# Choosing experts during a recurrence, four tiles at a time, in a fused attention and mixture-of-experts kernel

## The reference

```python
for t in range(S):                                   # attention, B 4, H 8, S 768, D 48
    state = alpha[:, :, t, :, None] * state + k_t (outer) v_t
    y[:, :, t] = q_t @ state
x = y as (3072 tokens, 384)
logits = unit(x) @ unit(expert_emb).T / tau          # 8 experts
e = argmax(logits);  gate = softmax(logits)[e]
x = gate * (relu(x @ w1[e]) @ w2[e])                 # 384 -> 1024 -> 384, one expert per token
h = x @ w_in;  g = max(0.01 * h, h)                  # 384 -> 2048
out = g @ w_out                                      # 2048 -> 384
```

## Time and profile before

| | |
|---|---|
| median of 3 runs | 880.02 us (879.15 to 881.05) |
| profiled execution | 880.55 us |
| its span, first to last instruction | 878.7 us |
| TensorE busy | 836.8 us, 95% |
| VectorE, ScalarE, GpSimd busy | 419.7, 334.2, 160.1 us |
| mean granted TensorE clock | 0.973 of full |

### The profile page before, as it was taken

One profiled execution on the slowest core, in us unless ns is written; L12 is line 12 of the kernel. 1 busy time (PEld: TensorE's weight loads), 2 busy tenths in 40 slices (PEclk: granted clock), 3 DMA queues, 4 the chain that ended last, 5 costly groups with the idle time before them and its releaser, 6 DMA issues.

```text
span 878.7 us, 17061 instructions
## 1 busy us (share of the span) xinstructions
PE 836.8 (95%) x5435; PEld 751.6 (86%) x5436; DVE 419.7 (48%) x643; ACT 334.2 (38%) x624; POOL 160.1 (18%) x216
## 2 busy tenths in 40 slices
PE   7999974899999999999997999999999999999998
PEld 6888854699999999999985999998998999999997
DVE  7788849444455253455244343343343343343332
ACT  2455443334435344444333333333333333333323
POOL 5566623222222222322210000000000000000000
PEclk7999995899999999999998999999999999999999
DMA  9898860552453351553305000200200300100100
GB/s 220 200 215 207 198 207 0 180 180 65 159 179 123 103 179 32 192 179 105 106 2 107 1 1 25 49 1 6 66 0 0 72 0 0 37 1 1 37 1 36
DMA packets 45265, 76.24 MB, mean 87 GB/s; under 512 B 16231, under 2 KB 35731, under 8 KB 45232
## 3 DMA queue, kind: packets, MB, share of 16 engines
q1 hardware_dynamic: 41264, 64.98, 26.6%
q0 software_dynamic: 3968, 10.82, 3.5%
HBM read 61.63 MB, written 15.53 MB: 88 GB/s over the span
## 4 chain that ended last, share of the span: by engine, by line
PE 84%; issue 4%; DVE 4%; POOL 3%; DMA 2%; SPq 1%; ACT 0%; POOLq 0%; DVEq 0%
PE bank L1326 23%; PE bank L1319 23%; PE bank L1269 15%; PE bank L1249 14%; PE bank L1260 3%; POOL kt L522 1%; PE bank L1240 1%; DVE decay L788 1%; PE bank L1148 1%; PE bank L1133 1%; PE bank L1168 1%; DMA xg<-x_rows,isrc 1%; DVE inv L796 1%; POOL state L530 1%; DMA taus<-tau 1%
## 5 line engine op out<-in xcount | busy, mean ns | idle before, releaser
L1319 PE MATMUL bank<-yT,wts 128*128 128x512 f32 x864 | 217.0, 396 | 6.1 <-DVE yT L1082 6.1
L1326 PE MATMUL bank<-wts,gs 128*128 128x384 f32 x1152 | 217.3, 337 | 0.0
L1326 PEld LDWEIGHTS bank<-wts,gs 128*128 128x128 f32 x1152 | 204.4, 188 | 8.9 <-issue 0.4
L1319 PEld LDWEIGHTS bank<-yT,wts 128*128 128x128 f32 x864 | 161.9, 189 | 36.6 <-DVE yT L1082 6.9
L1100 DVE TENSOR_TENSOR g<-bank,small 128x512 f32<-128x512 f32 x96 | 66.4, 691 | 180.6 <-ACT small L743 180.6
L1249 PE MATMUL bank<-wts,gxT 128*128 (+1 forms) x558 | 143.2, 401 | 1.2 <-DVE gxT L1037 1.2
L1269 PE MATMUL bank<-wts,hT 128*128 x744 | 137.3, 339 | 1.6 <-DVE hT L1053 1.6
L1269 PEld LDWEIGHTS bank<-wts,hT 128*128 128x128 f32 x744 | 128.5, 188 | 1.9 <-issue 1.8
L743 ACT ACTIVATE small<-bank 128x512 f32<-128x512 f32 x96 | 57.3, 597 | 191.0 <-PE bank L1319 190.9
L1249 PEld LDWEIGHTS bank<-wts,gxT 128*128 128x128 f32 x558 | 103.0, 190 | 20.9 <-DVE gxT L1037 1.5
L1102 DVE TENSOR_TENSOR gs<-g,gs 128x512 fp32r<-128x512 f32 x96 | 66.4, 692 | 67.0 <-ACT gs L746 67.0
(11 more groups left out here) (155 smaller groups left out, 676.9 us busy)
## 6 DMA issues: line engine op xcount, KB each, us to landing
raw<-w SPq DMA_DIRECT2D x14, 1536.0 KB, 7.1
qkas<-qka SPq DMA_DIRECT2D x40, 289.5 KB, 4.8
vs<-v SPq DMA_DIRECT2D x24, 192.0 KB, 4.7
x_rows<-xs SPq DMA_DIRECT2D x24, 192.0 KB, 4.5
yl<-y_rows SPq DMA_DIRECT2D x24, 192.0 KB, 4.4
out<-os SPq DMA_DIRECT2D x5, 768.0 KB, 4.3
raw<-w_in SPq DMA_DIRECT2D x2, 1536.0 KB, 6.8
raw<-w_out SPq DMA_DIRECT2D x2, 1536.0 KB, 7.3
```

The source lines that it names most:

```text
L1319: m = pe.matmul(gps[f % 2][:, :], wts[:, 0, w_part, n:n + P], yT[:, u, y_part, k], start=(k == 0 and (w_part, y_part) == (0, 0)), stop=(k ...
L1326: m = pe.matmul(ops[tt], gs[:, f % 4, g_part, tt * P:(tt + 1) * P], wts[:, 1, w_part, f * D:(f + 1) * D], start=(f == 0 and (g_part, w_par ...
```

## The change

The loops of the recurrence are written out. After every four tiles (two and two for the last four) VectorE chooses the experts (`route`), TensorE adds up the ranks (`rank_group`) and VectorE turns them into places (`rank`): the place of a token is 3072 times its expert's number plus its rank. GpSimd then scatters the token numbers of one tile with an indirect DMA of 4 byte elements to the DRAM tensor `lists` (`list_ids`), which SyncE filled with the number 3072 (nobody) at the start. The one-hot products and the slot tables are gone.

After 16 tiles one expert must have at least 256 tokens. It is picked (`choose_first`), its weights are loaded first, and its first two blocks come first; the order of experts is rotated to begin with it. GpSimd reads 128 numbers of the list with a DMA, waits for them and gathers with them (`read_ids`, `fetch`), for two blocks in step 21 and for every later block in `take_rows`. Four columns of numbers are used in turn, so reading one waits for the scatter of the block four before. `lay_out` makes the table of blocks while the first two blocks are under way. The gates are worked out after them (`weigh`) and are applied at the end, as the scale of ScalarE's output copy; `take_y` copies `ys` unscaled. Tile n is now row block n of `x_rows`, and the output is written back in the order of the reference. `SURE` is 4, `TILES` 24, `BATCHES` 4, `CH` 6. On VectorE `link` makes the next instruction wait for the one just issued.

```diff
+        GROUP_AT = {BATCHES * (g + 1) + 1: g for g in range(CH - 1)}
...
+            sp.wait_ge(tables_made, 1)
+            sp.dma_start(lists.rearrange("(p n) a -> p (n a)", p=P), nobody[:, :]).then_inc(lists_clear, 16)
...
+                refill_qka(n + 2)
+                if n == TILES - BATCHES - 2:
+                    sp.wait_ge(first_known, 1)
+                    expert0 = sp.value_load(est[0:1, 0:1], min_val=0, max_val=E - 1)
+                if n >= TILES - BATCHES - 2:
+                    load_first(2 * (n - TILES + BATCHES + 2), expert0)
+                    load_first(2 * (n - TILES + BATCHES + 2) + 1, expert0)
...
+            load_first(4, expert0)
+            load_first(5, expert0)
...
+            def list_ids(n, groups):
+                pool.wait_ge(pos_ready, groups)
+                pool.indirect_dma_start(
+                    out=lists, out_offset=bass.IndirectOffsetOnAxis(ap=posi[:, n:n + 1].bitcast(U32), axis=0),
+                    in_=token[:, n:n + 1], in_offset=None, bounds_check=E * CAP - 1, oob_is_err=False).then_inc(id_stored, 16)
...
+            def wait_stored(tiles):
+                pool.wait_ge(id_stored, 16 * tiles)
+                for s in x_stored:
+                    pool.wait_ge(s, 16 * tiles // BATCHES)
...
+            def read_ids(at, j, number):
+                pool.dma_start(members[:, j:j + 1], lists[ds(at, P)]).then_inc(members_in, 16)
+                pool.wait_ge(members_in, number * 16)
                 pool.sem_inc(pool_turns, 1)
...
-            def gather(w, u, n):
-                copy_index(n, isrc, slot_src, w, u)
+            def fetch(j, rows):
+                u = j % 2
                 pool.indirect_dma_start(
-                    out=xg[:, u, :], out_offset=None, in_=x_dram,
-                    in_offset=bass.IndirectOffsetOnAxis(ap=isrc[:, u:u + 1].bitcast(U32), axis=0),
-                    bounds_check=N - 1, oob_is_err=False).then_inc(gathered[u], 16)
...
+                    out=xg[:, u, :], out_offset=None, in_=x_dram[0:rows],
+                    in_offset=bass.IndirectOffsetOnAxis(ap=members[:, j:j + 1].bitcast(U32), axis=0),
+                    bounds_check=rows - 1, oob_is_err=False).then_inc(gathered[u], 16)
...
+            for n in range(TILES):
+                if n + 2 < TILES:
+                    prepare(n + 2)
...
+                if n == SURE * BATCHES + 5:
+                    wait_stored(SURE * BATCHES)
+                    pool.wait_ge(first_known, 1)
+                    expert0 = pool.value_load(est[0:1, 0:1], min_val=0, max_val=E - 1)
+                    for w in range(2):
+                        read_ids(expert0 * CAP + w * P, w, w + 1)
+                        fetch(w, EARLY)
+                if late == 0:
+                    pool.wait_ge(tables_made, TABLES)
+                    pool.wait_ge(lists_clear, 16)
+                if 0 <= late < TILES - BATCHES - 2:
+                    list_ids(late, late // BATCHES + 1)
+                if n == TILES - 2:
+                    list_ids(late + 1, CH - 1)
+                    list_ids(late + 2, CH - 1)
+                if 0 < n <= TILES - BATCHES:
+                    scale_state(n - 1)
+            for n in range(TILES - BATCHES, TILES):
+                list_ids(n, CH + (n - TILES + BATCHES) // 2)
+            wait_stored(TILES)
...
+            def take_rows(w, j, number):
+                at = pool.value_load(wlist[0:1, ds(w, 1)], min_val=0, max_val=E * CAP - P)
+                read_ids(at, j, number)
+                fetch(j, N)
...
-            def step(w, u, nxt, nxt2):
-                nxt3 = not isinstance(w, int) or w + 3 < WINDOWS
+            take_rows(2, 2, 3)
+            def step(w, j, first, nxt3):
                 if nxt3:
                     pool.wait_ge(gx_turned, w + 2)
-                    gather(w + 3, 1 - u, w * 2 + 4)
-                wait_scattered(pool, w, u, pool_turns)
-                copies = w * 2 + 5 if nxt3 else WINDOWS + 1 + w
-                copy_index(copies, idst, slot_dst, w, u)
+                    if not first:
+                        wait_scattered(pool, w + 1, 1 - j % 2)
+                    take_rows(w + 3, (j + 3) % IDS, w + 4)
                 pool.wait_ge(ys_ready, w + 1)
                 pool.sem_inc(pool_turns, 1)
                 pool.indirect_dma_start(
-                    out=y_dram, out_offset=bass.IndirectOffsetOnAxis(ap=idst[:, u:u + 1].bitcast(U32), axis=0),
-                    in_=ys[:, u, :], in_offset=None, bounds_check=N - 1, oob_is_err=False).then_inc(scattered[u], 16)
...
+                    out=y_dram, out_offset=bass.IndirectOffsetOnAxis(ap=members[:, j:j + 1].bitcast(U32), axis=0),
+                    in_=ys[:, j % 2, :], in_offset=None, bounds_check=N - 1, oob_is_err=False).then_inc(scattered[j % 2], 16)
...
+                if n >= FIRST_HI:
+                    split_hi(act, 0, 0, [n - FIRST_HI])
...
+            def route(g):
+                tiles = group_tiles(g)
...
+                dve.wait_ge(lg_copied, tiles[-1] + 1)
+                dve.tensor_reduce(lg, lgq[:, r0:r0 + G], AX.X, ALU.add).then_inc(lg_summed, 1)
...
+                last = len(group_tiles(g - 1)) if g > 0 else 0
+                source = sums[last][:, :, last] if g > 0 else carry[:, :]
+                dve.tensor_copy(heads[G][:, :, 0], source)
+                dve.wait_ge(lg_summed, g + 1)
+                link(dve.tensor_reduce(top, lg, AX.X, ALU.max))
+                link(dve.tensor_tensor(some, lg, over(top), ALU.is_equal))
+                link(dve.tensor_tensor(some, some, prio[:, :].unsqueeze(1).to_broadcast([P, G, E]), ALU.mult))
+                link(dve.tensor_reduce(most, some, AX.X, ALU.max))
+                link(dve.tensor_tensor(heads[G][:, :, 1:].rearrange("p e c -> p c e"), some, over(most), ALU.is_equal))
+                dve.tensor_tensor_scan(flat(sums[G][:, :, :]), flat(marks[G][:, :, :]), flat(heads[G][:, :, :]), 0.0,
+                                       ALU.mult, ALU.add).then_inc(hot_ready, 1)
+            def rank(g):
+                tiles = group_tiles(g)
+                G, n0 = len(tiles), tiles[0]
+                if g < SURE:
+                    dve.wait_ge(tile_done, BATCHES * (g + 1) + 2)
+                else:
+                    dve.wait_ge(rank_ready, g - SURE + 1)
+                ranks = rankps(g == CH)[:, 0:E * G].rearrange("p (e c) -> p e c", e=E)
+                dve.tensor_tensor(hits[G][:, :, :], ranks, heads[G][:, :, 1:], ALU.mult).then_inc(ranked, 1)
+                dve.wait_ge(ranked, g + 1)
+                link(dve.tensor_reduce(best[:, 0:G], hits[G][:, :, :].rearrange("p e c -> p c e"), AX.X, ALU.add))
...
+            def choose_first():
...
+                dve.wait_ge(counts_ready, 1)
+                link(dve.tensor_tensor(have, countps(False), ebase[:, 0, :], ALU.subtract))
+                dve.sem_inc(counted, 1)
+                link(dve.tensor_reduce(most, have, AX.X, ALU.max))
+                link(dve.scalar_tensor_tensor(out=chance, in0=have, scalar=most, in1=prio[:, :],
+                                              op0=ALU.is_equal, op1=ALU.mult))
+                link(dve.tensor_reduce(lead, chance, AX.X, ALU.max))
+                dve.tensor_scalar(est[:, :], lead, -1.0, float(E), ALU.mult, ALU.add).then_inc(first_known, 1)
+            def lay_out():
...
+                dve.wait_ge(first_known, 1)
+                expert0 = dve.value_load(est[0:1, 0:1], min_val=0, max_val=E - 1)
...
+                dve.wait_ge(counts_ready, 2)
+                link(dve.tensor_tensor(wend[:, :], countps(True)[0:1], ebase[0:1, 0, :], ALU.subtract))
...
+                link(dve.tensor_reduce(at, wprod[:, :, :], AX.X, ALU.add))
+                dve.scalar_tensor_tensor(out=wlist[:, :], in0=at, scalar=begin[:, 0:1], in1=wrow[:, :], op0=ALU.add,
+                                         op1=ALU.add).then_inc(tables_ready, 1)
+                link(dve.tensor_reduce(expert, wexp[:, :, :], AX.X, ALU.add))
...
+                link(dve.scalar_tensor_tensor(out=code, in0=second, scalar=4.0 * E, in1=code, op0=ALU.mult, op1=ALU.add))
+                dve.tensor_copy(wtab[:, :], code).then_inc(tables_ready, 1)
...
+            def weigh():
...
+                dve.wait_ge(exp_done, 1)
+                link(dve.tensor_reduce(gsum[:, :], ex[:, :, :], AX.X, ALU.add))
+                link(dve.tensor_scalar(gsum[:, :], gsum[:, :], 1e-9, None, ALU.add))
+                link(dve.reciprocal(gate[:, TG:], gsum[:, :]))
...
+            def take_y(w, u):
+                wait_scattered(dve, w, u)
+                dve.wait_ge(ye_ready, w + 2)
+                dve.tensor_copy(ys[:, u, :], yeps).then_inc(ys_ready, 1)
...
+                if n in GROUP_AT:
+                    route(GROUP_AT[n])
+                if n < TILES - BATCHES:
+                    advance(n)
+                if n in GROUP_AT:
+                    rank(GROUP_AT[n])
+                if n == SURE * BATCHES + 1:
```

(71 more changed lines are left out.)

836 lines of the change are left out of this document (355 added, 481 removed).

## The result

The kernel after takes **960.63 us** (median of 4 runs, 959.36 to 962.76), the kernel before, run beside it, 880.06. The ratio is 1.0918 (95% interval 1.0895 to 1.0941): slower, as forecast, but by 80 us in place of 24, and far outside the range of 876 to 926. The profiled execution has a span of 957.8 us, 79.1 more than before.

What follows compares the result with a forecast made beforehand. TensorE bounds the expert and dense stages, a ring of state, decay, reciprocal, inv and kt the recurrence. 36.2 - 2 + 5.0 - 17.4 + 2 = +23.8 on a span of 878.7 gave 904 us; 8-in-10 range 876 to 926.

Steps and rivals of the forecast that it cites:

- Block loop: Expert blocks: the longer chain from scatter through list read to gather nearly fits the 9.55 us rhythm; +2 us (0 to +17).
- rival 3: Block loop: a list read taking 1 us more makes GpSimd's list set the block; 15 more, 919 us; chance 0.16.
- Gap: From R to block 2's second product: R + 46 in place of R + 63.4, -17.4 us (-12; at most -31).
- R: End of the last recurrence matmuls, 127.4 us before the change; forecast 17.0 us after decay of tile 23.
- Early gather: End of recurrence: TensorE waits for the first gather ahead of tile 22's projection, delaying R by 5.0 us (2 to 9).
- TensorE may come back slow: Between recurrence and blocks: after a pause of 5.4 us TensorE may run at a lower clock; 2 us added.
- Recurrence: Recurrence tiles: 12 steps with a scatter at 1.15 us and 4 choice steps at 5.6 us more, +36.2 us.
- the queue order is what costs here: Choice steps 5, 9, 13, 17: GpSimd waits for VectorE's positions, then decay for GpSimd; 10.3 us, 5.6 over the period.
- Loops written out: Recurrence: register arithmetic saved, 0.1 us in each of 20 steps, -2 us (0 to -4).
- gates: Dense stage: scaling on ScalarE's output copy is covered by TensorE; 0 us, or 2.4 without cover.
- Rival 1: Recurrence: decay need not wait for state, so scatters and waits fall into GpSimd's idle time; 868 us; chance 0.15.
- Rival 2: Recurrence: each scatter holds GpSimd 1.75 to 1.95 us, partly from a 1.66 us gather; 9.6 more, 913 us; chance 0.15.

Runs made afterwards that it cites:

- ids8_ahead: Changed kernel with eight columns of token numbers in place of four, and each block's list read issued one block ahead: 918.43 us.
- ids8: Changed kernel with eight columns of token numbers in place of four, so a list read waits for an older scatter (block w-5, not w-1): 929.90 us.
- light_loads: Changed kernel with the second to eighth expert's weights left out but for a twelfth of each (result not computed): 920.00 us.
- late_loads: Changed kernel with the second expert's weight load started only when all token numbers have landed in the lists: 957.11 us.
- shift: Changed kernel with every token number scattered one step later, still between kt and the state product: 956.10 us.
- behind: Changed kernel with the token scatter put after scale_state on GpSimd, waits as they were: 945.44 us.
- comb_split_turn: ids8_ahead plus token scatters later and behind the state product, state sum signalled before rank products, ranks a step later, first early gather turned after the last tile: 902.35 us.

## Why the forecast was wrong

**Block loop, +2 in place of +42.8: the term that failed.** The step was "scatter to landing 2.7" in GpSimd's list of 9.2 us, of 9.55 available, read off the last scatter of the kernel. The mechanism was there, the room (0.35 us) was there, and rival 3 named the consequence; only it hung the doubt on the list read, which took less than the 2.7 given to it (2.3 us in the median), and gave the whole case 17 us. What failed is one landing taken for all: those beside a weight load took 4.0 to 6.3. In the seven pairs the first took 5.9 us on average and the second 4.3. Against 2.7 each, and less the room of two blocks, that is 4.1 us a pair or 29 in all (an estimate from these landings); TensorE's waits for gathered rows add up to 27.1. The rest is its clock: it was busy 288.2 us in this stage and 274.5 in ids8_ahead, which has the same products. ids8 and light_loads show both halves of the cause: take the wait away, or the bytes, and 29 us go.

**Gap, -17.4 in place of -6.2.** Block 0's second product started at R + 22.0 (R + 20.2 forecast). The last scatter landed at R + 28.5 and not at R + 16: 3 us of that are a later start (its positions were made at R + 14.1, not 10.9), 9 its landing of 12.1 where 2.7 was taken. It is the same mistake a second time: an unloaded landing in a stretch in which the weights of the second expert are loaded. Without most of them (light_loads) block 2 comes at R + 45.3, against R + 46, and the chain there runs through VectorE's `lay_out` and `weigh`, as forecast. With the load only put off (late_loads, R + 52.2) the weights are late instead.

**Early gather, +5.0 in place of +7.3.** The size was near by luck, since the cause was another. 2.3 were for a wait; in the changed kernel there is none, because TensorE itself came 3.3 us late, at half clock after its wait for the choice. The forecast used this effect in the gap ("TensorE may come back slow") and not here, where a pause of 4 us stood in its own working.

**Recurrence, +34.2 against +34.0.** The terms: an ordinary step 5.89 (4.72 + 1.15 = 5.87), a choice step 9.6 to 10.0 (10.3), four table reads and conversions as written. The reason given for the choice steps was wrong, though. They were put down to GpSimd's order ("the queue order is what costs here"); shift, which takes that wait away, gained 1.3 us, since VectorE's list and TensorE's late `tile_done` were almost as long and stood behind it. The order of the two lines cost about 16 times a scatter (behind: 17.3). That the choice steps had the right length with the wrong reason was luck.

**Loops written out -2, gates 0.** Neither can be seen singly; the dense stage is 1.2 us longer.

**Rivals.** Rival 1 is out: each `decay` waits for `state`. Rival 2 is out in the recurrence: the scatters of numbers take 1.01 us in the median, and about 0.15 lie ahead of one. But the 1.66 on which it rested is a real effect. The longest scatter of numbers is the one beside VectorE's weight subtractions, which read two SBUF operands:

```profile
171.59 2.35 DVE L353 TENSOR_TENSOR wts<-raw,wts 128x1024 fp32r<-128x1024 f32 x2
172.01 1.64 POOL L554 DMA_INDIRECT lists<-token,posi  x1 [2.36 <-DVE posi L909]
```

Two scatters of rows beside such subtractions took 1.65 and 2.03 us, the other 29 at most 1.03. The Trainium skill, "SBUF — State Buffer", section "SBUF: two separate sides", says that a VectorE operation with two SBUF inputs holds up a GpSimd operation that reads SBUF. These rows agree; in the recurrence the scans and masks have one input in PSUM, and the scatters aren't held up.

Rival 3 had the right engine and the wrong transfer. The Trainium skill gives a fixed 2.0 us for such a small DMA ("DMA: Bandwidth & Descriptors", section "Anatomy of one DMA — SWDGE (gpsimd) path"). The shortest landing of a scatter of rows is 2.0 here, but the longest is 6.3 and the last scatter of numbers in comb_split_turn took over 16, so it is a floor and no price.

## What to carry to other kernels

Before a transfer that nothing waited for is put into a chain, price it beside the loads that will be in flight with it, and never by the last one, which runs alone. A median hides this as well: it was 2.7 in the changed kernel, where 14 of 31 took 4.0 to 6.3. The landing line of a tile's view is no help either, since it mixes every transfer that touches the tile: in the view of `y_rows` SyncE's 24 reads are counted with the scatters. If a list has 0.35 us of room, the spread of its terms decides, not their sum. A wait that keeps a buffer from being overwritten should look as far back as it can: two lines and four more columns were worth 30 us here. And a removed wait shows the next one in the queue: of the 4 us that GpSimd waited for positions, VectorE's list had nearly all.
